# Expert 0's slots loaded early, completed by one-hot matmuls; zeros on the tensor engine; ends reordered

## What is computed

```
mask   = argmax(q_n . c_n) == argmax(k_n . c_n)        # 16 clusters per head
attn   = softmax(where(mask, q k^T / 8, -1e9)) @ v     # -> x, 1536 tokens x 512
h      = x @ w_in                                      # 512 -> 2048
x      = (h * sigmoid(1.702 h)) @ w_out                # 2048 -> 512
noisy  = x @ w_gate + log1p(exp(x @ w_noise)) * noise  # 8 experts
top2   = the two largest, weights = softmax over them
out    = sum over the two: w_e * (relu(x @ w1[e]) @ w2[e])   # 512 -> 1024 -> 512
```

## Time and profile before

| | us |
|---|---|
| median of 3 runs | 946.74 (945.55 to 947.07) |
| the profiled execution | 947.12 |
| its span, first to last instruction | 945.3 |
| PE busy | 900.9 (95%) |
| DVE, ACT, POOL busy | 525.3, 420.4, 137.9 |
| mean granted clock of PE | 0.971 |

### The profile page before, as it was taken

How to read it: one execution, slowest core, us unless ns; L and a number is a source line. 1 busy time by engine, 2 the same in 40 slices (tenths; PEclk the granted TensorE clock), 3 DMA queues, 4 the chain that set the end, 5 groups by cost and what they waited for, 6 DMA issues and landing times.

```text
span 945.3 us, 12455 instructions
## 1 busy us (share of the span) xinstructions
PE 900.9 (95%) x4314; PEld 732.3 (77%) x4315; DVE 525.3 (56%) x949; ACT 420.4 (44%) x685; POOL 137.9 (15%) x144
## 2 busy tenths in 40 slices
PE   6999999999999999999999991999999999999995
PEld 4777777777766888888888881888888888888884
DVE  7787878888755443456345533445344443444373
ACT  4667777676774332352235230424344243424320
POOL 2021221222121000005000504100000000005072
PEclk7999999999999999999999995899999999999998
DMA  5132432333174222325332534325263453428364
GB/s 121 38 92 75 124 92 52 120 90 94 41 236 165 97 89 89 134 90 178 90 133 89 179 109 150 130 90 175 85 206 114 146 178 116 166 89 285 121 220 146
DMA packets 84301, 118.98 MB, mean 126 GB/s; under 512 B 19258, under 2 KB 47930, under 8 KB 84256
## 3 DMA queue, kind: packets, MB, share of 16 engines
q1 hardware_dynamic: 79328, 104.08, 34.2%
q0 software_dynamic: 4928, 14.35, 4.4%
HBM read 89.12 MB, written 29.39 MB: 125 GB/s over the span
## 4 chain that ended last, share of the span: by engine, by line
PE 86%; DVE 8%; issue 2%; DMA 2%; ACT 1%; POOL 1%; SPq 0%; POOLq 0%; DVEq 0%; ACTq 0%
PE psum L867 10%; PE psum L868 10%; PE psum L869 10%; PE psum L881 9%; PE psum L783 9%; PE psum L882 9%; PE psum L883 9%; PE psum L748 3%; PE psum L768 3%; PE psum L769 3%; PE psum L1012 2%; DVE neg_max L1364 2%; PE psum L879 1%; PE psum L878 1%; PE psum L725 1%
## 5 line engine op out<-in xcount | busy, mean ns | idle before, releaser
L783 PE MATMUL psum<-probs,vx 128*128 128x386 f32 x384 | 155.8, 487 | 0.3 <-ACT probs L1078 0.3
L881 PE MATMUL psum<-down_hi,hid_hi 128*128 128x512 f32 x384 | 151.3, 394 | 0.0
L882 PE MATMUL psum<-down_lo,hid_hi 128*128 128x512 f32 x384 | 149.8, 390 | 0.0
L883 PE MATMUL psum<-down_hi,hid_lo 128*128 128x512 f32 x384 | 149.8, 390 | 0.0
L1243 ACT ACTIVATE hid_hi<-psum 128x448 fp32r<-128x448 f32 x64 | 34.8, 544 | 185.5 <-PE psum L869 185.5
L1078 ACT ACTIVATE probs<-psum 128x384 f32<-128x384 f32 x192 | 90.2, 488 | 54.9 <-PE psum L769 52.9
L1364 DVE TENSOR_REDUCE neg_max<-psum 128x1 f32<-128x768 f32 x96 | 91.3, 955 | 24.4 <-PE psum L748 20.7
L1646 DVE SCALAR_TENSOR_TENSOR hid_lo<-psum,hid_hi 128x384 fp32r<-128x384 f32 x64 | 35.6, 557 | 124.0 <-ACT hid_hi L1243 124.0
L1217 ACT ACTIVATE gelu<-psum 128x512 f32<-128x512 f32 x48 | 28.7, 598 | 158.9 <-PE psum L869 158.9
L867 PE MATMUL psum<-sx_hi,up_hi 128*128 128x448 f32 x256 | 94.7, 370 | 0.0
L868 PE MATMUL psum<-sx_lo,up_hi 128*128 128x448 f32 x256 | 94.5, 369 | 0.0
(11 more groups left out here) (194 smaller groups left out, 1495.1 us busy)
## 6 DMA issues: line engine op xcount, KB each, us to landing
raw<-in_moe_w SPq DMA_DIRECT2D x64, 512.0 KB, 4.3
raw<-in_moe_w_in SPq DMA_DIRECT2D x24, 512.0 KB, 3.4
raw<-in_moe_w_out SPq DMA_DIRECT2D x24, 512.0 KB, 5.1
slot_x<-zeros SPq DMA_DIRECT2D x7, 1024.0 KB, 5.5
slot_rows<-slot_x SPq DMA_DIRECT2D x8, 768.0 KB, 5.3
raw_q<-in_q SPq DMA_DIRECT2D x30, 192.0 KB, 3.4
raw_k<-in_k SPq DMA_DIRECT2D x30, 192.0 KB, 3.7
slot_y<-y_sb SPq DMA_DIRECT2D x7, 768.0 KB, 3.8
```

What stands on the lines that cost most here:

```text
L783: mm(psum[:, 5 + half, 0:WIDE], vx[:, n % 2, c], probs[:, at % SLOTS], start=(c == 0), stop=(c == J - 1)).then_inc(unit_done, 1)
L881: mm(dst, hid_hi[:, f % 2, cols], down_hi[:, slot, f % GP], start=(f == 0), stop=False)
L882: mm(dst, hid_hi[:, f % 2, cols], down_lo[:, slot, f % GP], start=False, stop=False)
L883: return mm(dst, hid_lo[:, f % 2, cols], down_hi[:, slot, f % GP], start=False, stop=(f == pieces - 1))
```

## The change

Five things are done.

1. SP loads expert 0's slots during chunk 2, after the scatters of chunks 0 and 1. POOL waits for that load before chunk 2's scatters. Chunk 2's own rows for expert 0 aren't read back: PE puts the loaded slots into psum with matmuls by `ident` (`kept_slots`) and adds, in the same psum groups, `y_sb`'s rows (as `row_hi` + `row_lo`, in space of `xt_hi` and `xt_lo` that is free by then) times one-hot matrices (`moves`), which DVE makes by comparing the slot number with a row 0 to 447.
2. Eight `idle_rows` stand ahead of this on PE.
3. Loads of the slots of experts 1 to 7 stand behind two of four weight groups.
4. In the last head DVE splits group 0, then does `head_result`, then splits group 1.
5. In expert 7, `ORDER` is 0, 3, 1, 2 and `down_end` covers pieces 5 to 7 tile by tile; piece 7 has a hidden buffer of its own.

```diff
-        ORDER = (FULL,) + tuple(range(FULL))
+        ORDER = (0, FULL) + tuple(range(1, FULL))
+        def row_hi(j):
+            return xt_hi[:, j, 0:CT]
+        def row_lo(j):
+            return xt_lo[:, j, 0:CT]
+        def moves(j):
+            return xt_hi[:, j, CT:CT + CAP]
...
-            keep_rows(t)
...
+            sp.wait_ge(scattered_low, (CHUNKS - 1) * (DMA * TPC))
+            load_slots(0, 0)
+            keep_rows(t)
...
-                    when(sx_done, n * DC + DC)
-                    load_slots(r, e + 1)
                     for i in range(EGR):
+                        if i == STAGES:
+                            when(sx_done, n * DC + DC)
+                            sp.wait_ge(scattered_low, DMA * TILES)
+                            sp.wait_ge(scattered, DMA * TILES)
+                            load_slots(r, e + 1)
                         load_group(weights_of(e + 1, i), EXPERT0 + n * EGR + i + RING, i % STAGES)
...
-            sp.wait_ge(scattered_low, DMA * TILES)
-            load_slots(0, 0)
-            sp.wait_ge(scattered, DMA * TILES)
...
+            with pool.Fori(0, CHUNKS - 1) as t:
+                scatter_chunk(t)
+            chain.link(nc.gpsimd.iota(slot_i[:], pattern=[[1, CAP]], base=-FAR, channel_multiplier=0))
+            nc.gpsimd.tensor_copy(slot_of[:], slot_i[:]).then_inc(slot_of_set, 1)
+            pool.wait_ge(sx_in, 2 * DMA)
+            scatter_chunk(CHUNKS - 1)
...
-            def down_end(f, slot, piece, pieces):
...
+            def down_end(piece0, pieces):
+
                 for i, j in enumerate(ORDER):
+                    for f in range(pieces - 3, pieces):
+                        if i == 0:
+                            pe.wait_ge(hid_done, piece0 + f + 1)
+                        last = down_tile(f, f // GP % RING, True, j, pieces, 2 if f == pieces - 1 else None)
+                        if i == YT - 1 and f % GP == GP - 1:
+                            last.then_inc(group_used, 1)
+                    if i < YT - 1:
                         last.then_inc(y_ready, 1)
...
-                    if f >= 1:
+                    if f >= 1 and not (end and f == pieces - 2):
                         down(f - 1, ((f - 1) // GP) % RING, rest, piece0 + f - 1, pieces)
...
                 for f in range(TPC):
                     logits(p, f, f, LAST)
+                pe.wait_ge(sx_in, 2 * DMA)
+                idle_rows(8, FULL)
+                for c in range(DC // 2):
+                    kept_slots(c)
                 ranks(p, LAST)
+                for c in range(DC // 2, DC):
+                    kept_slots(c)
+                for c in range(DC):
+                    move_rows(c)
+
+            def kept_slots(c):
+
+                for j in range(YT):
+                    rows = rows_of(j)
+                    mm(psum[:, turn_bank(c, True), j * P:j * P + rows], slot_rows[0:rows, j, c * P:(c + 1) * P],
+                       ident[0:rows, 0:rows], start=(j == 0), stop=False)
+
+            def move_rows(c):
+
+                dst = psum[:, turn_bank(c, True), 0:CAP]
+                for j in range(TPC):
+                    if c == 0:
+                        pe.wait_ge(split_lo, j + 1)
+                        pe.wait_ge(moves_ready, j + 1)
+                    mm(dst, row_hi(j)[:, c * P:(c + 1) * P], moves(j), start=False, stop=False)
+                    last = mm(dst, row_lo(j)[:, c * P:(c + 1) * P], moves(j), start=False, stop=(j == TPC - 1))
+                last.then_inc(sx_turned, 1)
...
+                act.wait_ge(y_act, LEAD + 2 * p + 2)
+                act.wait_ge(y_dve, LEAD + 2 * p + 2)
+                for j in range(TPC):
+                    copy(row_hi(j), y_sb[:, j], ACT.Copy).then_inc(split_hi, 1)
                 softplus(p, LAST)
...
-                    for x in range(4):
-                        split(0, x // 2, x % 2)
+                    for part in range(2):
+                        split(0, 0, part)
...
                 head_result(n, 0)
+                if n == HEADS - 1:
+                    for part in range(2):
+                        split(0, 1, part)
...
+                for j in range(TPC):
+                    dve.wait_ge(split_hi, j + 1)
+                    dv.tensor_tensor(row_lo(j), y_sb[:, j], row_hi(j).bitcast(F32), ALU.subtract)\
+                        .then_inc(split_lo, 1)
                 select(p, at, chain, LAST)
-                place(p, at, chain, LAST)
+                first_moves(p, chain, LAST)
+                def turn_half():
+
+                    for c in range(DC // 2):
+                        turn_lo(0, c, True)
+
+                place(p, at, chain, LAST, turn_half)
+                for c in range(DC // 2, DC):
+                    turn_lo(0, c, True)
+
+            def first_moves(p, chain, held):
+
+                chain.link(dv.scalar_tensor_tensor(out=key[:, 0], in0=r_one[:, 0, :, 0], scalar=-float(FAR),
+                                                   in1=base[:, 0:1].broadcast_to((P, TPC)), op0=ALU.mult, op1=ALU.add))
+                dve.wait_ge(slot_of_set, 1)
+                dve.wait_ge(rank_ready, p + 1)
+                chain.link(dv.tensor_tensor(
+                    key[:, 1], psum[:, held, RANK0:RANK0 + TPC * E].rearrange("p (j e) -> p j e", e=E)[:, :, 0],
+                    key[:, 0], ALU.add))
+                for j in range(TPC):
+                    dv.tensor_scalar(moves(j), slot_of[:], key[:, 1, j:j + 1], None, ALU.is_equal)\
+                        .then_inc(moves_ready, 1)
...
                 dve.sem_inc(slots_ready, 1)
+                if between:
+                    between()
```

More of the change, by code:

```diff
@@ L626, in _, with scatter_chunk @@
             pool.wait_ge(cleared, ALL_CLEARED)
-            with pool.Fori(0, CHUNKS) as t:
+            def scatter_chunk(t):
                 when(slots_ready, LEAD + t + 1)
@@ L870, in up, with down_tile @@
                 last.then_inc(hid_ready, 1)
-            def down_tile(f, slot, rest, j, pieces):
+            def down_tile(f, slot, rest, j, pieces, held=None):
+                held = f % 2 if held is None else held
                 dst = bank(j)
                 if rest and j == FULL:
-                    both = hid_hi[:, f % 2, j * P:]
+                    both = hid_hi[:, held, j * P:]
                     mm(dst, both, down_hi[:, slot, f % GP], start=(f == 0), stop=False)
@@ L880, in down_tile @@
                 cols = slice(j * P, (j + 1) * P)
[L881 to L883 removed]
+                mm(dst, hid_hi[:, held, cols], down_hi[:, slot, f % GP], start=(f == 0), stop=False)
+                mm(dst, hid_hi[:, held, cols], down_lo[:, slot, f % GP], start=False, stop=False)
+                return mm(dst, hid_lo[:, held, cols], down_hi[:, slot, f % GP], start=False, stop=(f == pieces - 1))
             def down(f, slot, rest, piece, pieces):
@@ L1022, in experts @@
             def experts(r, end):
-                turn_slots(r * E, 0, True)
-                turn_slots(r * E, 1, True)
+                if not end:
+                    turn_slots(r * E, 0, True)
+                    turn_slots(r * E, 1, True)
                 with pe.Fori(0, E - 1) as e:
@@ L1242, in expert_step @@
                     act.wait_ge(hid_ready, PIECE0 + n * (FE // P) + f + 1)
-                    copy(hid_hi[:, f % 2, 0:CAP], psum[:, 4 + f % 2, 0:CAP], ACT.Relu).then_inc(hid_act, 1)
+                    held = 2 if end and f == FE // P - 1 else f % 2
+                    copy(hid_hi[:, held, 0:CAP], psum[:, 4 + f % 2, 0:CAP], ACT.Relu).then_inc(hid_act, 1)
                     splits(m0, f, FE // P, last=last)
@@ L1493, in route, with turn_lo @@
                     place(p, at, chain, 6)
+            def turn_lo(n, c, first=False):
+                dve.wait_ge(sx_act, n * DC + c + 1)
+                dv.tensor_tensor(sx_lo[:, c], psum[:, turn_bank(c, first), 0:CAP], sx_hi[:, c].bitcast(F32), ALU.subtract)\
+                    .then_inc(sx_done, 1)
             def route_last(p, chain):
@@ L1534, in select, with place @@
                 dv.tensor_tensor(r_sel[:], r_one[:, 0], r_one[:, 1], ALU.add).then_inc(sel_ready, 1)
-            def place(p, at, chain, held):
+            def place(p, at, chain, held, between=None):
                 dve.wait_ge(rank_ready, p + 1)
@@ L1643, in expert_step @@
                     dve.wait_ge(hid_act, PIECE0 + n * (FE // P) + f + 1)
-                    for lo, cols in ((hid_lo[:, f % 2, 0:FULL * P], slice(0, FULL * P)),
-                                     (hid_hi[:, f % 2, CAP:], slice(FULL * P, CAP))):
+                    held = 2 if after and f == FE // P - 1 else f % 2
+                    for lo, cols in ((hid_lo[:, held, 0:FULL * P], slice(0, FULL * P)),
+                                     (hid_hi[:, held, CAP:], slice(FULL * P, CAP))):
                         last_lo = dv.scalar_tensor_tensor(out=lo, in0=psum[:, 4 + f % 2, cols], scalar=0.0,
```

(7 more changed lines are left out.)

33 lines of the change are left out of this document (13 added, 20 removed).

## The result

The changed kernel took **936.92 us**, median of 4 runs (934.88 to 937.95), beside 946.9 for the kernel before (945.55 to 949.09): ratio 0.9895, 95% interval 0.9874 to 0.9917. It is faster by 10 us where I had forecast 19.6, and it lies 3.4 us outside the range. Beside later experiments the same kernel took 930.38 us in another group of runs (ratio 0.9827, interval 0.9811 to 0.9844). Nearly all of the difference between the two, 6.2 of 6.5 us, is one thing, which the experiments are about. The first profiled execution took 937.32 us (span 935.5), the one of the other group 930.77 (span 929.0).

The account below looks back on a forecast made before the run. TensorE was taken as the bound, so changes pay only where it idles or runs at 1.2 GHz, with POOL's queue setting the end. 3.9 + 13.4 + 2.3 = 19.6 us gave 927.2 us, range 924.5 to 933.5.

Parts of the forecast that it names:

- Seam: Attention to chunk 0: PE's wait for head 15 (2.2 us) and the half clock after it (1.7 us) go; gain 3.9 us.
- PE idle in chunk 0: Sign of being wrong: PE idle before piece 2 of chunk 0, which needs group 1's splits, reckoned 0.4 us later.
- Bridge: Last routing, chunk 2's end to expert 0: unbroken PE queue starts expert 0 at 584.0, full clock; gain 13.4 us.
- only the load of expert 1's slots waits for that: Routing: POOL's last scatters, through near 594, hold up nothing but that load.
- Slots of experts 1 to 7: Loaded behind two weight groups; expert 1's land near 601, before they are wanted; cost nothing.
- End: Expert 7's last pieces: POOL's output scatters no longer queue, last starts at 935.8 instead of 938.10; gain 2.3 us.
- The four scatters I had wanted with holes between them: Sign in the last three microseconds: holes between output scatters; back to back would mean POOL still bounds.
- the five: Rivals: half clock through bridge 0.15, PE held by handover 0.15, end gains nothing 0.08, early load late 0.02, slower 0.03.
- the handover that holds PE by 2 to 4 us: Rival in the bridge: one-hot tiles late, loads not hidden or lo tiles queued on DVE; about 930.5 us, chance 0.15.
- half clock bridge: Rival: half clock through the bridge, expert 0 starts at 590.0, gain 7.4 instead of 13.4; 933.2 us, chance 0.15.
- The rule of the Trainium skill: Transposes do not count as a busy PE; the bridge's plain matmuls and zeros would count towards full clock.
- the bound I had put at 1.6 better: Bridge: clock never falls, zeros cost 1.7 less, expert 0 starts at 582.4; gain 15.0 us.

Follow-up runs that it names:

- chip D: Group of four runs on one chip, one session: the changed kernel unaltered and three variants, no signal late; 928.55 to 930.38 us, kernel before 946.72.
- after_again: The changed kernel run again with nothing altered: 939.4 us, ratio 0.9918 to the kernel before.
- chip A: Group of four runs on one chip, one session: the changed kernel again and three variants, with late signals; 931.72 to 941.2 us, kernel before 946.97.
- slots_first: Changed kernel with SP asking for the slots of experts 1 to 7 ahead of the weight groups again: 937.18 us, ratio 0.9894 to the kernel before.
- chip B: Group of four runs on one chip, one session: last chunk's scatters delayed or paced, seam or end change alone; 930.91 to 947.27 us, kernel before 947.46.
- peeled_third: Changed kernel with ScalarE's expert 0 written out ahead of its loop, scatters 12 in a row: 928.29 us, ratio 0.9795 to the kernel before.
- peeled_second: Changed kernel with ScalarE's expert 0 written out ahead of its loop, in another group: 929.01 us, ratio 0.9816 to the kernel before.
- after_third: The changed kernel, nothing altered, in another group of runs: 930.38 us, ratio 0.9827 to the kernel before.
- no_last_scatters: Changed kernel without POOL's 12 scatters of the last chunk: 931.72 us, ratio 0.9837 to the kernel before.
- held scatters: Changed kernel with POOL waiting, ahead of the last chunk's scatters, until VectorE finished piece 2 of expert 0: 932.44 us, ratio 0.9841 to the kernel before.
- seam_alone: Kernel before with only VectorE's reordered splits in the last head: 944.26 us, ratio 0.9970 to the kernel before.
- end_alone: Kernel before with only the change at the end: 947.27 us, ratio 0.9991 to the kernel before.

## Why the prediction was off, step by step

**Seam: the mechanism was right, the size 3.0 instead of 3.9 us.** The hole (2.5 us for 2.2) and the half clock went as worked out. Not reckoned: with no hole ahead of it, piece 0's hid_lo, made of gelu and 1.39 us of DVE (twice its usual 0.69, while POOL's xt_lo, started 0.37 us earlier, takes 1.21 beside it), holds PE, a spacing of 1.07 us instead of 0.23; and chunk 0's first matmul takes 0.3 us more. 1.67 - 0.84 - 0.31 = 0.5, and 0.4 to 0.5 was measured. I had named PE idle in chunk 0 as what would show the step wrong, and looked for it at piece 2 only.

**Bridge: right in every term where no signal is late.** Zeros 3.4 us at half clock (3.39), the first kept_slots 2.1 (2.6, begun at half clock), move_rows 6.5 (6.58), slots 3.2 us later, the last one-hot tile 0.4 us ahead of its first matmul; expert 0 at 20.4 us behind chunk 2's end where I had 20.0. On chip D 12.8 of 13.4 us came.

**The step that failed** is one sentence of that part: of POOL's scatters, "only the load of expert 1's slots waits for that". They cost nothing in the sum. In the kernel before they lay beside a PE that stood idle for 16.4 us; now they lie beside expert 0, where every piece needs a signal from PE to ScalarE and on to DVE. By the first profile piece 0 has 1.1 us to spare for that (2.2 us late, PE waits 1.13) and a later piece some 3.6. Where signals come late while POOL issues, that cost 4.0 us in the first profile (59.18 against 55.14) and 6.3 in after_again, with the clock's fall. The same lateness took 1.5 us of expert 6 and 0.7 of the end: 4.0 + 1.5 + 0.7 = 6.2 of the 6.5 us between the first profile after and that of chip D; the last 0.3 are in the stretches ahead. Of the 9.8 us by which the first profile misses the forecast of 19.6, then, 6.2 are late signals, 1.8 the stretch up to attention's end and the other 1.8 terms of seam and bridge that came out somewhat smaller.

**Slots of experts 1 to 7: nothing, where no signal is late** (42.4 us each). On chip A the new order went with the 1.5 us of expert 6, as slots_first shows.

**End: 2.15 of 2.3 us** on chip D, 1.5 in the first profile, where PE's stall was 0.90 instead of 0.25. Alone, on chip B, it couldn't be told from nothing by the times. The four scatters I had wanted with holes between them follow each other after 0.30 to 0.46 us on chip D, so POOL has next to nothing in hand there, and a still earlier PE would win little.

**What I left at zero, the stretch up to attention's end,** was 1.6 to 1.8 us longer in both profiles after. Attention's last matmul starts between 285.2 and 289.2 us in the 17 traces with the changed bridge, and between 285.6 and 286.8 in the three without; the spread is there at the first of its matmuls, before 30 us. Whether that is chance stays open.

**The rivals.** None of the five is what happened; the nearest is the handover that holds PE by 2 to 4 us, but it named the bridge's own handovers, and those were in time. The clock was full from early in kept_slots on, DVE kept up, SP's loads were no wait. My range reached to 933.5 for a half clock bridge, and a time of 930.4 lies in it; 936.9 does not, since no case of mine had a signal late. The rule of the Trainium skill I had leant on ("TensorE: Matmul & The Clock Gate", Part 4) was not put to a test of its own. It fits that with zeros and plain matmuls in the transposes' place the half clock lasted 3.4 us in 13 of the 15 traces that have both, and 10.2 without the zeros. It doesn't say why in peeled_third half clock lasted 6.8 us and the bridge took 21.9, nor why in peeled_second the clock never fell behind the same transposes.

**What is shown and what is not.** Shown: the waits belong to some chips or sessions, or their recording, and not to the kernel alone (after_third); on such a chip expert 0's need the scatters (no_last_scatters against after_again); and it is PE's increments that are recorded late, with ScalarE 0.02 us behind them. Shown less firmly, since the changed kernel did not run on chip B: scatters in pairs or 15 us later free expert 0 there, while signals elsewhere in the same traces stay late. Open: why an increment of PE takes effect late. Every time of this study comes from an execution that was recorded, and lateness and missing records always come together. The Trainium skill ("NOTIFIC — the notification-queue block", 7.1) says that the block which writes such records can discard them when its ring is full and that its internal pipeline holds back the engines that feed it; no run here shows that this is what happened, and a time without recording was not to be had. ScalarE's entry into its loop has no need to be brought in: no kernel with it written out met late signals, but the records of PE's increments put the delay ahead of ScalarE.

## What to carry to other kernels

When an edit closes a hole, list what used to run beside the hole: here 12 scatters lost an idle PE as their cover and got a chain of short handovers instead. Pacing such a burst in pairs cost nothing that could be measured on chip D, and on chip B, where other signals were late, neither the paced nor the held scatters made expert 0 wait. And before a difference between kernels is called a cause, look in both traces at a place that the edit did not touch: it was expert 6 that showed two groups of runs to be on different ground.

## What I had not expected of the hardware

- The same kernel has two times by group of runs, 936.9 to 939.4 and 930.4 us, with the durations of instructions alike; the kernel before has nearly one (946.97 and 947.46 against 945.26 to 946.73).
- A late signal comes while POOL issues a row of 12 or 16 indirect DMAs and mostly ends 0.7 to 1.9 us after the last of them: in expert 6 of the first profile the last gather is issued at 864.21 + 0.95 = 865.16 and hid_hi starts at 866.63. But the first one of expert 0 ends within the row, and so does expert 6's in slots_first, seam_alone and end_alone. Other counts, from DVE to PE and from ScalarE to DVE, were on time in between.
- PE's holes of 3.3 us in after_again and 3.45 in slots_first were each followed by half clock for about 3.4 us; one of 2.6 us in the first profile was not. In peeled_second the same transposes and 16-column matmuls never lost full clock, and the bridge took 18.9 us instead of 20.4, the bound I had put at 1.6 better.
